# Sums of the attention probabilities in two column groups of 64 with three sources, without VectorE's addition of the last two tiles

## The reference

```python
q_pool = q.reshape(B, H, S // factor, factor, D).mean(axis=3)
scores = scale * np.matmul(q_pool, k.transpose(0, 1, 3, 2))
scores = scores - np.max(scores, axis=-1, keepdims=True)
attn = np.exp(scores)
attn = attn / (np.sum(attn, axis=-1, keepdims=True) + 1e-09)
return np.matmul(attn, v).astype(np.float32)
```

## Time and profile before

| | |
|---|---|
| median of 3 runs | 743.3 us (743.18 to 743.6) |
| span of the profiled execution | 738.7 us |
| PE busy | 724.9 us, 98% of the span |
| PEld (weight loads) busy | 540.5 us, 73% |
| DVE busy | 523.4 us, 71% |
| POOL busy | 485.1 us, 66% |
| ACT busy | 455.6 us, 62% |
| mean granted TensorE clock | 0.995 of 2.4 GHz |

### The profile page before, as it was taken

How to read it: one execution, slowest core, us unless ns; L and a number is a source line. 1 busy time by engine, 2 the same in 40 slices (tenths; PEclk the granted TensorE clock), 3 DMA queues, 4 the chain that set the end, 5 groups by cost and what they waited for, 6 DMA issues and landing times.

```text
span 738.7 us, 17096 instructions
## 1 busy us (share of the span) xinstructions
PE 724.9 (98%) x6375; PEld 540.5 (73%) x6375; DVE 523.4 (71%) x826; ACT 455.6 (62%) x1008; POOL 485.1 (66%) x431
## 2 busy tenths in 40 slices
PE   7999999999999999999999999999999999999997
PEld 5776777777777777777777677434778888888886
DVE  6888888888888888888888847533894555455542
ACT  3677776776777767767767763214655454545453
POOL 2588888888888888888888873212774444444442
PEclk8999999999999999999999999999999999999999
DMA  5123335334244353353342347899301010101011
GB/s 142 47 59 100 106 95 157 99 111 151 88 120 143 91 155 105 98 164 88 112 151 88 96 140 259 298 387 387 132 1 43 1 43 0 43 0 43 0 43 43
DMA packets 51623, 81.83 MB, mean 111 GB/s; under 512 B 14556, under 2 KB 20572, under 8 KB 51548
## 3 DMA queue, kind: packets, MB, share of 16 engines
q1 hardware_dynamic: 51468, 80.69, 35.0%
q10 hardware_dynamic: 80, 0.13, 0.0%
HBM read 75.94 MB, written 4.79 MB: 109 GB/s over the span
## 4 chain that ended last, share of the span: by engine, by line
PE 93%; DVE 3%; ACT 1%; issue 1%; POOL 1%; DMA 0%; SPq 0%; DVEq 0%; POOLq 0%; ACTq 0%
PE ps L680 20%; PE ps L657 8%; PE ps L987 8%; PE ps L986 8%; PE ps L985 8%; PE ps L625 6%; PE ps L659 5%; PE ps L661 5%; PE ps L663 5%; PE ps L691 3%; PE ps L585 3%; PE ps L975 2%; PE ps L899 2%; PE ps L869 2%; PE ps L590 1%
## 5 line engine op out<-in xcount | busy, mean ns | idle before, releaser
L1072 ACT ACTIVATE probs<-ps 128x576 f32<-128x576 f32 x288 | 183.8, 652 | 44.0 <-PE ps L663 28.9
L1356 DVE TENSOR_REDUCE mx<-ps 128x2 f32<-128x1024 f32 (+1 forms) x160 | 189.2, 1217 | 29.1 <-PE ps L625 27.1
L551 POOL TENSOR_TENSOR g_lo<-g_buf,g_hi 128x384 fp32r<-128x384 f32 x96 | 102.1, 1066 | 100.8 <-ACT g_hi L1245 100.8
L680 PE MATMUL ps<-probs,v_sb 128*64 128x288 f32 x1152 | 146.8, 409 | 0.1
L512 POOL TENSOR_TENSOR p_sum<-p_sum,probs 128x576 f32<-128x576 f32 x93 | 129.1, 1413 | 0.0
L1584 DVE SCALAR_TENSOR_TENSOR v_buf<-u_buf 128x384 f32<-128x384 f32 x96 | 60.2, 627 | 86.7 <-ACT u_buf L1238 86.1
L680 PEld LDWEIGHTS ps<-probs,v_sb 128*64 128x64 f32 x1152 | 79.7, 137 | 56.3 <-issue 5.2
L1238 ACT ACTIVATE u_buf<-ps,half 128x384 f32<-128x384 f32 x96 | 55.8, 582 | 93.7 <-PE ps L975 93.7
L985 PE MATMUL ps<-wo_hi,g_hi 128*128 128x512 f32 x282 | 110.5, 392 | 0.6 <-POOL g_lo L551 0.4
L987 PE MATMUL ps<-wo_lo,g_hi 128*128 128x512 f32 x282 | 110.8, 393 | 0.0
L986 PE MATMUL ps<-wo_hi,g_lo 128*128 128x512 f32 x282 | 110.6, 392 | 0.0
(11 more groups left out here) (214 smaller groups left out, 1251.6 us busy)
## 6 DMA issues: line engine op xcount, KB each, us to landing
pre<-in_moe_w SPq DMA_DIRECT2D x41, 512.0 KB, 4.7
k_raw<-in_k SPq DMA_DIRECT2D x32, 288.0 KB, 3.8
v_sb<-in_v SPq DMA_DIRECT2D x32, 288.0 KB, 2.8
q_raw<-in_q SPq DMA_DIRECT2D x32, 256.0 KB, 3.9
from_x<-in_moe_w SPq DMA_DIRECT2D x9, 512.0 KB, 5.2
p_inv<-inv_dram SPq DMA_DIRECT2D x62, 72.0 KB, 2.6
out<-o_stage SPq DMA_DIRECT2D x34, 128.0 KB, 2.4
staged<-in_moe_w SPq DMA_DIRECT2D x8, 512.0 KB, 5.2
```

What stands on the lines that cost most here:

```text
L680: mm = pe.matmul(ps[D * h:D * h + D, 4, 0:HALF], v_sb[n % 2][:, u, :], probs[:, u, HALF * h:HALF * h + HALF], start=(i == 0), stop=(i == N ...
L1072: nc.scalar.activation(dst, ps[:, b0:b0 + 2, 0:HALF], ACT.Exp, scale=SCORE_SCALE).then_inc(exp_done, 1)
L1356: top = nc.vector.tensor_reduce(mx[0:w, NC * t:NC * t + 2], ps[0:w, b:b + 2, :], AX.X, ALU.max)
```

## The change

For heads 0 to 30, `add_up` multiplies ones with three sources in the order tile 6, tile 7, `p_sum`, each in two halves of 288 columns, on column groups of 64 (6 products of 288 columns for 8 of 144). It writes to columns 0 to 287 of bank 5 and waits for `probs_added` ahead of the third source. `add_pair` and the waits for it are gone. `read_x` takes 288 columns of bank 5 for 144 of bank 4, so `x_sum` is 128 x 288, and the DMA that spreads it reads two partitions (0 and 64) with 288 values each for four with 144. In the last head, the first product with `phi` (which writes bank 5) waits for the last `read_x`.

```diff
-    QUAD = SQ // 4
...
-    x_sum = at("x_sum", [P, QUAD], 65536)
+    x_sum = at("x_sum", [P, HALF], 73984)
...
-                             x_sum[0:P:SLOTS, :].rearrange("c (p j) -> c p j", j=NT)).then_inc(sums_spread, 16)
+                             x_sum[0:P:D, :].rearrange("c (p j) -> c p j", j=NT)).then_inc(sums_spread, 16)
...
             def add_up(n):
 
                 if n + 1 < HEADS:
-                    pe.wait_ge(probs_added, ADDS * n + ADDS)
-                    pe.wait_ge(pair_added, n + 1)
-                    for src, first in ((p_sum[:, :], True), (probs[:, NT - 2, :], False)):
-                        for c in range(4):
-                            mm = pe.matmul(ps[SLOTS * c:SLOTS * c + SLOTS, 4, HALF:HALF + QUAD], ones[:, 0:SLOTS],
-                                           src[:, QUAD * c:QUAD * c + QUAD], start=first, stop=not first)
+                    for i, src in enumerate((probs[:, NT - 3, :], probs[:, NT - 2, :], p_sum[:, :])):
+                        if i == 2:
+                            pe.wait_ge(probs_added, ADDS * n + ADDS)
+                        for h in range(2):
+                            mm = pe.matmul(ps[D * h:D * h + D, 5, 0:HALF], ones[:, :],
+                                           src[:, HALF * h:HALF * h + HALF], start=(i == 0), stop=(i == 2))
                 else:
                     pe.wait_ge(probs_added, ADDS * n + LAST_ADDS)
-                    pe.wait_ge(pair_added, n + 3)
+                    pe.wait_ge(pair_added, 3)
...
                     if n == HEADS - 1 and s == 3:
                         pe.wait_ge(phi_loaded, 16)
+                        pe.wait_ge(x_read, HEADS - 1)
                         logits(0, range(0, KD // 2))
...
                     else:
-                        act.wait_ge(pair_added, n)
                         act.wait_ge(sums_done, n)
...
                 nc.scalar.activation(x_raw[n % 2][:, :], ps[:, 4, 0:HALF], ACT.Copy)
-                nc.scalar.activation(x_sum[:, :], ps[:, 4, HALF:HALF + QUAD], ACT.Identity,
+                nc.scalar.activation(x_sum[:, :], ps[:, 5, 0:HALF], ACT.Identity,
                                      bias=eps[:, :]).then_inc(x_read, 1)
...
-            def add_pair(n):
-                dve.wait_ge(exp_done, NT * n + NT)
-                dve.wait_ge(pv_done, NT * n + 1)
-                nc.vector.tensor_tensor(probs[:, NT - 2, :], probs[:, NT - 2, :], probs[:, NT - 3, :],
-                                        ALU.add).then_inc(pair_added, 1)
...
-                if n + 1 < HEADS:
-                    add_pair(n)
-                else:
+                if n + 1 == HEADS:
                     top_logits(0)
                     add_last(n)
```

More of the change, by code:

```diff
@@ L1390, in add_last @@
                 for i, u in enumerate((NT - 3, NT - 2)):
-                    dve.wait_ge(pair_added, n + 1 + i)
+                    dve.wait_ge(pair_added, 1 + i)
                     nc.vector.tensor_tensor(p_rest[:, :], p_rest[:, :], probs[:, u, :], ALU.add).then_inc(pair_added, 1)
```

## The result

The changed kernel takes 766.76 us (median of 4 runs, 765.97 to 767.79), the kernel before 743.45 us beside it (4 runs, 743.18 to 743.97). The ratio is 1.0322 with a 95% interval of 1.0304 to 1.0341: **slower by 3.2%**, 23.3 us. The forecast was 768.7 us, with a range of 764.4 to 774.4.

A forecast was written before the change was run, and what follows sets the result against it. TensorE, busy for 98% of the span, was taken to bound the kernel. Its added 25.4 us on the 738.7 us span gave 764.1, and 4.6 us to the median gave 768.7 us; range 764.4 to 774.4.

The forecast's parts named there:

- TensorE's stream: TensorE at each head's end: 5.97 us for 5.15, 0.82 us more per head, +25.4 us over 31 heads.
- The change-over saved: Products with the values, no longer followed by four groups of 32, take 4.41 us for 4.52, saving 0.11 per head.
- VectorE's addition at nothing: Removing VectorE's 1.91 us pair addition per head gains nothing, being covered by `weigh` and the ones product.
- The rival without it: Change-over at the head's end not saved: 28.8 to 30.1 us added, 772.1 to 773.4 us; chance 0.17.
- GpSimd's addition at nothing: GpSimd's last addition per head shortens from 1.80 to 1.41 us, but TensorE gains nothing.
- ScalarE's second copy: At the head's end, 288 columns take 0.41 us for 0.38 with 144; counted as nothing, 1 us to the upper end.
- The rival in which waits for exponentials swallow the delay: TensorE's waits in the scores absorb up to 21.5 of the 25.4 us, giving 747.2 us; chance 0.03.
- The ones product hidden: Rival at the head's end: ones product hidden beneath `weigh`, VectorE setting L625's start; 20 us gained, 723 us; chance 0.02.
- The spreading DMA: DMA after the copies, from two partitions: 2.0 us of slack, costing nothing; rival that it is late, chance 0.01.
- The step from the span to the median: Whole-kernel time: the median's 4.6 us above the page's span was added to 764.1 us, giving 768.7.

The follow-up runs named there:

- pair added: Changed kernel with VectorE's addition of the pair put back: two sources in two column groups of 64; 755.28 us for 742.71, ratio 1.0158 against the kernel before.
- 144 columns: Kernel before with two column groups of 64, only 144 columns each, half of the sums left out; 737.62 us for 742.71, ratio 0.9933.
- three sources: Kernel before without VectorE's addition, with tile 6, tile 7 and `p_sum` as sources in four groups of 32; 749.59 us for 742.71, ratio 1.0107.
- no addition: Kernel before with `add_pair` and its waits taken out, so the sums leave out tile 6; 742.70 us for 742.71, ratio 1.0003.
- second copy: Kernel before with one more ScalarE copy of 288 columns between the two of `read_x`, result unread; 742.99 us for 743.16, ratio 0.9998.
- the second addition: Kernel before with another VectorE addition of 432 columns ahead of that of the pair, result unread; 785.00 us for 743.16, ratio 1.0575.
- a fourth source: Changed kernel with `p_sum` taken as a source twice; 782.63 us for 743.16 of the kernel before, ratio 1.0541.

## Why the prediction was right

- **TensorE's stream, +25.4 us.** Right, in its parts as well: 4.41 + 0.97 + 0.59 = 5.97 us per head, and 25.4 us over the stretch.
- **The change-over saved.** Right: 4.41 to 4.42 us in the kernels in which the ones product has two groups of 64 (the changed one, pair added, 144 columns), 4.51 to 4.52 with four groups of 32 (before, three sources, no addition, second copy). The rival without it is out; the run with 144 columns shows the 0.11 us by themselves.
- **VectorE's addition at nothing.** Right, shown by taking it out alone: 1.0003. Its idle time came out in two places, 0.78 us ahead of the subtractions and 2.68 ahead of the maxima, for the 3.6 that I put ahead of the maxima; the subtractions can't move up by the whole 1.9 us, since they need ScalarE's roundings. But the cover was 0.28 us, thinner than its 1.91 us of work suggests, and the second addition shows what lies behind: some 1.4 us per head.
- **GpSimd's addition at nothing.** Right; 1.42 us as forecast.
- **ScalarE's second copy.** Its size was wrong: 0.50 us for the 0.41 that I took from the copy of 288 columns beside it. The second copy adds a bias with another function, so the copy beside it was not its like; which of the two makes the difference was not tried. It cost nothing: the first exponential still starts 1.07 us after L624 (321.87 - 320.80), as before.
- **The rival in which waits for exponentials swallow the delay.** Out: 21.4 us after, and 21.9 with a fourth source.
- **The ones product hidden.** Out: each source shows its 0.49 us, also with a fourth.
- **The spreading DMA.** VectorE waits for it once, in the last head, as before.
- **The step from the span to the median.** This term of the sum was mis-sized, and the forecast is 1.9 us too high for it. I took the 4.6 us between the page's span and the median for a constant; in the changed kernel it is 766.76 - 764.2 = 2.6 us. In its timed runs, device time is 1.8 us over the span of the same execution (765.97 over 764.2), so the rest is how the profiled execution compares with the timed ones. That of before was a quick one: its 738.7 us and 1.8 make 740.5, below all four timed runs beside the changed kernel (743.18 to 743.97) and near the lowest of those timed later (740.9). The changed kernel was profiled in one of its two quicker runs of four. The stretch gives +25.4 us and the medians +23.3, with 22.6 to 25.4 as the interval. Starts and ends that differ by up to 3.4 and 1.2 us between traces can make up such a difference, but the share of each is not shown.

## What to carry to other kernels

Where TensorE streams without a gap, price an edit from start to start of its rows, and look for the new form elsewhere in the same trace: here the last head had it, and gave the cost per source and the change-over to 0.01 us. VectorE's addition had only 0.3 us of cover, and still it saved TensorE a source of 0.24 us in the old form and 0.48 in the new one and cost nothing: work on an engine counts for nothing as long as what it releases is not late, and so does taking it away. Measure such a cover by adding work, from start to start, before leaning on it. Don't add the distance between one page's span and the median to a forecast as if it were fixed. Look at how an execution starts, too: executions of programs that are the same up to there differed by 3 us, more than many an edit is worth.

## What was not expected

- The change from products of 128 x 64 to products of 128 x 32 costs the stream 0.11 us (4.52 for 4.41), and leaves the weight loads standing 0.4 us, although both use all 128 rows.
- VectorE's 432-column addition took 1.78 us beside GpSimd's additions, where one of 576 columns took 0.84 us alone. Two additions in a row paid this each (1.78 and 1.96). The other way round it is shown: GpSimd's addition falls from 1.80 to 1.41 us when VectorE's is taken out. That VectorE's is slow for GpSimd's is argued from the rows; no run took GpSimd's away.
- TensorE ran at half its pace up to 26 us in some executions and at full pace from 20 us in others, and in two of the slow ones the granted clock of the view read 1.00. 27 more dummy transposes in the first 20 us were worth 1.8 us.
